# Top-32 attention feeding a gated product on one core: groups of 128 tokens, weights as the moving operand, and the hidden tile turned on TensorE

## The reference, cut to what matters

```
scores = (q @ k.T) / sqrt(64)              # 4 batches, 8 heads, 576 x 576
kth    = 32nd largest of each row
scores = where(scores >= kth, scores, -1e9)
attn   = softmax(scores)                   # sum + 1e-9
x      = (attn @ v) -> [2304 tokens, 512]
out    = ((x @ w_a) * (x @ w_b)) @ w_out   # w_a, w_b: 512 x 1536, w_out: 1536 x 512
```

## Time and profile before

| | |
|---|---|
| median of 3 executions | 875.44 us |
| the profiled execution | 875.8 us, span 874.0 us |
| busy PE, weight loads, DVE, ACT, POOL | 814.9, 734.0, 780.9, 623.4, 455.5 us |
| granted TensorE clock, mean | 0.969 |
| moved by DMA | 81.48 MB, mean 93 GB/s |

### The profile page before, as it was taken

One profiled execution on the slowest core, in us unless ns is written; L12 is line 12 of the kernel. 1 busy time (PEld: TensorE's weight loads), 2 busy tenths in 40 slices (PEclk: granted clock), 3 DMA queues, 4 the chain that ended last, 5 costly groups with the idle time before them and its releaser, 6 DMA issues.

```text
span 874.0 us, 19133 instructions
## 1 busy us (share of the span) xinstructions
PE 814.9 (93%) x6576; PEld 734.0 (84%) x6576; DVE 780.9 (89%) x1663; ACT 623.4 (71%) x1416; POOL 455.5 (52%) x504
## 2 busy tenths in 40 slices
PE   6666679999999999999999999999999999999997
PEld 4455568889899998898899999898999998898996
DVE  7899999998999999999999999999999999995000
ACT  5787777777877777778777777787777777775222
POOL 2677754555544455555554455655445445544332
PEclk9966689999999999999999999999999999999999
DMA  4635552222522232224422322233323222311332
GB/s 124 152 110 164 194 164 56 75 75 75 147 80 68 73 97 74 73 80 128 107 77 73 91 68 74 73 106 89 95 74 103 68 68 68 91 55 56 109 91 85
DMA packets 133520, 81.48 MB, mean 93 GB/s; under 512 B 82736, under 2 KB 110384, under 8 KB 133424
## 3 DMA queue, kind: packets, MB, share of 16 engines
q1 hardware_dynamic: 132880, 80.12, 33.0%
q10 hardware_dynamic: 544, 0.13, 0.1%
HBM read 70.78 MB, written 9.44 MB: 92 GB/s over the span
## 4 chain that ended last, share of the span: by engine, by line
DVE 51%; PE 31%; issue 10%; ACT 4%; POOL 2%; DMA 1%; SPq 0%; ACTq 0%
DVE work L904 25%; DVE best L887 20%; PE ps L536 12%; PE ps L551 6%; DVE keep L919 6%; PE ps L462 3%; PE ps L501 3%; PE ps L484 2%; PE ps L420 2%; POOL scores L810 2%; PE ps L434 1%; ACT scores L670 1%; ACT q_t L635 1%; DMA k_rows_b<-in_k 1%; PE ps L442 0%
## 5 line engine op out<-in xcount | busy, mean ns | idle before, releaser
L887 DVE MAX8 best<-work 128x8 f32<-128x576 f32 x432 | 304.7, 747 | 0.0
L536 PE MATMUL ps<-x_hi,w_hi 128*128 128x256 f32 x864 | 251.4, 291 | 0.9 <-ACT x_lo L688 0.9
L810 POOL TENSOR_TENSOR scores<-scores,keep 128x576 f32<-128x576 f32 x144 | 214.7, 1510 | 58.5 <-DVE keep L919 58.5
L536 PE MATMUL ps<-x_lo,w_hi 128*128 128x256 f32 x864 | 243.2, 281 | 0.0
L904 DVE MATCH_REPLACE8 work<-best,work 128x576 f32<-128x576 f32 x288 | 212.8, 743 | 0.0
L536 PE MATMUL ps<-x_hi,w_lo 128*128 128x256 f32 x648 | 182.4, 281 | 0.0
L536 PEld LDWEIGHTS ps<-x_hi,w_hi 128*128 128x128 f32 x864 | 163.0, 189 | 2.2 <-ACT x_lo L688 1.4
L820 POOL TENSOR_TENSOR h_lo<-ab,h_hi 128x256 fp32r<-128x256 f32 x108 | 81.0, 750 | 158.5 <-ACT h_hi L699 158.5
L536 PEld LDWEIGHTS ps<-x_lo,w_hi 128*128 128x128 f32 x864 | 163.2, 189 | 0.5
L655 ACT ACTIVATE scores<-scores,neg_max 128x576 f32<-128x576 f32 x144 | 111.9, 778 | 68.0 <-POOL scores L810 67.2
L462 PE MATMUL ps<-k_t,q_t 128*128 128x288 f32 x632 | 121.2, 320 | 4.9 <-ACT scores L643 4.9
(11 more groups left out here) (56 smaller groups left out, 1294.4 us busy)
## 6 DMA issues: line engine op xcount, KB each, us to landing
wo_lo<-x_scratch SPq DMA_DIRECT2D x108, 256.0 KB, 2.7
wb_lo<-x_scratch SPq DMA_DIRECT2D x108, 128.0 KB, 2.2
stage<-in_w SPq DMA_DIRECT2D x36, 256.0 KB, 3.0
q_rows<-in_q SPq DMA_DIRECT2D x142, 64.0 KB, 2.3
x_scratch<-wo_lo SPq DMA_DIRECT2D x18, 256.0 KB, 2.8
v_rows<-in_v SPq DMA_DIRECT2D x32, 128.0 KB, 2.4
out<-stage SPq DMA_DIRECT2D x15, 256.0 KB, 2.7
k_rows_a<-in_k SPq DMA_DIRECT2D x16, 128.0 KB, 2.3
```

Of the source, the lines that this page charges most:

```text
L536: last = mm(ps_ab[:, which, :], w, x[:, g % 2, kb, :], start=(kb == 0 and i == 0), stop=(kb == KB - 1 and i == 2))
L810: V.tensor_tensor(row, row, keep[:, j, :], ALU.add).then_inc(mask_done, 1)
L887: ins = V.max(best[:, u % 2, j, 8 * r:8 * r + 8], src)
```

## The change

The group becomes 128 tokens, so there are 18, each with 4 chunks of 384 hidden columns: 72 chunks n, and one of them is started in each slot from slot 5 (n = s - 5), the last slot being 78. x is now stationary and the weights move, 384 columns at a time: 12 matmuls for a and 12 for b, the product with tokens on the partitions. The product of the two therefore has to be turned by PE (`turn_hidden`, three transposes) before it can be the stationary operand of the output. ACT copies the turned h out of PSUM twice, the high part and the whole, and POOL subtracts. In POOL's list the subtraction (`hidden_lo`) of chunk n-2 stands behind the masks and shifts of slot s, that is one slot after the copies. The output product (9 matmuls of 512 columns) is made in two steps, six matmuls from h's high part at the start of the slot, three from its low part later. Each of the two products has a PSUM bank of its own; before, both shared one. The low parts of the output weights are read 768 KB at a time in one buffer, those of w_b 384 KB at a time in one buffer, where before they were in rings of two. The weights are loaded in the order in which the chunks of columns need them, up to five in a slot, through four stages; their outgoing low parts have a tile of their own. The key parts are put in slots 13, 14, 15, 15, 16, 16, 17, 17; 30 to 37; 49, 50, 51, 51, 52, 52, 53, 53; the order of the query tiles changes in two batches, and v is loaded one slot earlier.

```diff
-    G = 256
-    GT = G // P
+    G = P
     GROUPS = TOKENS // G
+    HC = 384
+    HB = HC // P
+    NH = DFF // HC
+    NCH = GROUPS * NH
...
-    ORDER = [[0, 1, 2, 3, 4], [0, 4, 1, 2, 3], [0, 1, 2, 4, 3], [4, 0, 1, 2, 3]]
+    ORDER = [[0, 1, 2, 3, 4], [4, 0, 1, 2, 3], [0, 1, 2, 3, 4], [4, 0, 1, 2, 3]]
...
+        at = first_unit(b, 0)
+        PREP_SLOT += [at + n for n in ((-5, -4, -3, -3, -2, -2, -1, -1) if b % 2 else (-6, -5, -4, -3, -2, -1, 0, 1))]
...
     MOE0 = PER + 1
-    MOE_END = LAST
+    MOE_END = MOE0 + NCH + 2
...
+    STAGES = 4
+    W_AT = [(0, 2), (0, 4)] + [(1, m) for m in (0, 1, 2, 4)] + [(s, m) for s in range(2, 5) for m in range(5)]
+    W_AT += [(s, m) for s in range(5, 9) for m in (0, 1, 2, 4)]
...
+            def load_wo(n):
+                if not 0 <= n < NCH:
+                    return
+                wait(sp, o_done, n)
+                f = n % NH * HB
+                if n < NH:
+                    stored_until(W_ORDER.index(WO0 + f + HB - 1))
+                sp.dma_start(wo_lo[:].bitcast(fp32), xs_o[f * P:(f + HB) * P, :].rearrange("(b p) c -> p b c", p=P)
+                             ).then_inc(ld_wo, 16)
```

SP's loop:

```diff
+            for s in range(FIRST, MOE_END):
...
+                load_wo(n - 1)
+                load_q(s + 4)
+                for b, p in V_AT.get(s, []):
                     load_v(b, p)
+                if n >= 2 and (n - 2) % NH == NH - 1:
+                    store_y((n - 2) // NH)
...
+                load_wb(n + 1)
```

PE's three steps and its loop:

```diff
+            def columns_of(n, which, blocks):
...
+                if which == 0:
+                    wait(pe, xlo_done, PER * g + (3 if blocks[0] == 0 else PER))
+                for kb in blocks:
...
+                    for m, (x, w) in enumerate(((x_hi, high), (x_hi, low), (x_lo, high))):
+                        last = mm(ps_ab[which], x[:, g % 2, kb, :], w,
+                                  start=(kb == 0 and m == 0), stop=(kb == KB - 1 and m == 2))
...
+            def turn_hidden(n):
...
+                pe.wait_ge(h_ready, n + 1)
+                wait(pe, ht_copied, n)
+                for b in range(HB):
+                    last = tr(ps_h[:, b * P:(b + 1) * P], ab[:, 0, b * P:(b + 1) * P], ident[:])
...
+            def output(n, part):
...
+                    if part == 0:
+                        mm(ps_y, h_hi[:, cols], high, start=(f + b == 0), stop=False)
+                        mm(ps_y, h_hi[:, cols], wo_lo[:, b, :], start=False, stop=False)
+                    else:
+                        last = mm(ps_y, h_lo[:, cols], high, start=False, stop=(f + b == NF - 1))
...
+            for s in range(FIRST, MOE_END):
                 mine = preps_at(s)
+                n = s - MOE0
+                output(n - 2, 0)
                 probs_v(s - 2)
                 q_transposes(s + 2)
                 qk(s + 1, 0)
+                columns_of(n, 0, (0, 1))
+                output(n - 2, 1)
                 x_subtract(s - 2)
                 q_subtract(s + 2)
                 qk(s + 1, 1)
                 if mine:
                     wait(pe, qt_ready, min(s + 3, NU))
+                for m in mine:
+                    k_transposes(m)
+                columns_of(n, 0, (2, 3))
+                wait(pe, xlo_done, min(s - 1, NU))
+                turn_hidden(n - 1)
                 wait(pe, qt_ready, min(s + 3, NU))
                 wait(pe, kt_ready, parts_until(s))
                 transposes(s - 1, 0)
+                columns_of(n, 1, (0, 1, 2, 3))
                 transposes(s - 1, 1)
```

The second half of a slot on ACT:

```diff
                 normalise(s - 1, 0)
+                copy_y(n - 2)
                 x_out(s - 2, x_lo, xsub_done, xlo_done)
                 copy_q(s + 2, 1)
                 copy_scores(s + 1, 1)
+                for m in mine:
+                    copy_k(m)
                 normalise(s - 1, 1)
+                copy_hidden(n - 1)
+                weights(s, 2)
+                copy_ab(n, 0)
+                weights(s, 3)
                 copy_probs_t(s - 1, 0)
+                weights(s, 4)
+                copy_ab(n, 1)
                 copy_probs_t(s - 1, 1)
```

A slot on POOL:

```diff
                 masked(s - 1, 0)
                 masked(s - 1, 1)
                 shifts(s)
+                n = s - MOE0
+                hidden_lo(n - 2)
+                hidden(n - 1)
+                for m in range(2, 5):
+                    weights(s - 1, m)
+                weights(s, 0)
+                for m in [m for m in preps_at(s) if not split_early(m)] + [m for m in preps_at(s + 1) if split_early(m)]:
+                    split_k(m)
+                weights(s, 1)
```

More of the change, by code:

```diff
@@ L40, in topk_attention_gated_product @@
     WO0 = 2 * WB0
+    NCB = DFF // WC
     LOW = WO0 - 6
@@ L339, in load_wo @@
[L339 to L352, removed]
@@ L354, in store_y, with load_w @@
-            def store_y(g):
[L355 to L368, removed]
+            def load_w(i):
+                if i < WCH:
+                    wait(sp, w_lo_done, i - STAGES + 1)
+                    sp.dma_start(stage[:, i % STAGES, :], w_parts[W_ORDER[i]]).then_inc(ld_w[i % STAGES], 16)
@@ new lines, in stored_until @@
+            def stored_until(last):
+                for n in range(LOWS):
+                    wait(sp, st_w[n], 16 * sum(LEAVING[m] <= last for m in range(n, len(LEAVING), LOWS)))
+            def load_wo(n):
[7 more added lines that the diff above has]
+                             ).then_inc(ld_wo, 16)
@@ new lines, in load_wb @@
+            def load_wb(n):
+                if not 0 <= n < NCH:
+                    return
+                wait(sp, ab_done[1], n)
+                if n < NH:
+                    stored_until(W_BASE[columns_need(n) - 1] + KB - LKB - 1)
+                at = n % NH * HC
+                sp.dma_start(wb_lo[:].bitcast(fp32), xs_b[:, :, at:at + HC].rearrange("k p c -> p k c")
+                             ).then_inc(ld_wb, 16)
+            def store_y(g):
+                sp.wait_ge(y_ready, g + 1)
+                for at, n, row in PIECES[g]:
+                    sp.dma_start(out[row:row + n, :], y[at:at + n, g % 2, :]).then_inc(st_y, 16)
@@ L375, in _ @@
             load_q(2)
-            for c in range(STAGES):
-                load_w(c)
+            load_w(0)
+            load_w(1)
             load_k(4)
@@ L553, in step @@
+                if part == 1:
                     last.then_inc(o_done, 1)
-            def steps(todo):
-                for n in todo:
-                    step(n)
             pe.wait_ge(s_ident, 2)
@@ new lines, in copy_ab, with copy_hidden @@
+            def copy_ab(n, which):
+                if not 0 <= n < NCH:
+                    return
+                act.wait_ge(ab_done[which], n + 1)
+                if which == 0:
+                    wait(act, ht_done, n)
+                else:
+                    wait(act, h_ready, n)
+                A.copy(ab[:, which, :], ps_ab[which]).then_inc(ab_copied[which], 1)
+            def copy_hidden(n):
+                if not 0 <= n < NCH:
+                    return
+                act.wait_ge(ht_done, n + 1)
+                wait(act, o_done, n)
+                A.copy(h_hi[:], ps_h).then_inc(h_hi_ready, 1)
+                wait(act, h_lo_ready, n)
+                A.copy(h[:], ps_h).then_inc(ht_copied, 1)
```

395 lines of the change are left out of this document (161 added, 234 removed).

## The result

The changed kernel takes 867.5 us in the median (866.3 to 868.4) against 875.4, a ratio of 0.991 [0.989, 0.993]: 7.9 us less. The profiled execution took 866.3 with a span of 864.5. The forecast was 859, so the direction holds and the time lies in the range, but the gain is just under half of the 16.4 that was promised. The kernel before was timed again beside the experiments; its median lay between 874.6 and 875.4, so differences of about 1 us between medians of this document say nothing.

A forecast was written before the change was run, and what follows sets the result against it. The time was taken as the end of DVE's work (D, 798.1 us) plus what PE has left then (75.9). From the profiled 875.8, +5.5 in D and -22.0 behind it gave 859.3, taken as 859; range 847 to 880.

The forecast's parts named there:

- Slot on PE: PE's work in every slot: 10.47 us, 0.24 more than before, 0.09 under DVE's 10.56.
- Distance of matmuls: Start-to-start time of PE's 384-column matmuls: 0.176 us, the midpoint between 0.118 at 256 columns and 0.233 at 512.
- h's path: POOL's low part of h ends 3.8 us into DVE's slot, PE needs it 4.6 into its own: costed at nothing.
- The load: The 768 KB load of `wo_lo` takes 4.7 us: hidden by 0.5 in the slots, not in the tail.
- D: End of DVE's last mask, 798.1 us before: rises 5.5 to 803.6.
- Early slots: Slots 1 to 8, with POOL full in 5 to 8 and PE's clock partly low: adds 4 us (0 to 12).
- Keys: Slots with key parts and neighbours: about 20 have 0.24 less slack on PE, +5 us; 3.5 taken back for `keep`.
- Behind D: What PE has left after DVE's last mask: 53.9 us instead of 75.9, 22.0 less, with load-set slots of 7.9.
- PE as the bound of every slot: Rival: PE stalls exceed the 0.09 slack in each slot; 0.45 per slot costs 24 us, giving 883; chance 0.14.
- The load over 5.3 us: Rival: the `wo_lo` load outlasts its cover in the slots; at 6.2 it adds 60 us, about 919; chance 0.04.
- The gain going to D: Rival: first nine slots +12, keys +12, nothing back; D rises 21 us, time about 875; chance 0.09.
- The collisions of `keep` vanishing: Rival: these and the waits in key slots mostly vanish; D falls 5 us, time 848; chance 0.14.

The follow-up runs named there:

- late inversion: The changed kernel with DVE's inversion a round later, between the two removals of round 2: 866.8 us, ratio 0.991.
- left-out matmuls: The changed kernel without two of each chunk's three output matmuls with h's low part, so part of the product is missing: 849.4 us, ratio 0.973.
- early release: The changed kernel with the next `wo_lo` load issued after the six high output matmuls, not after the three low ones: 859.7 us, ratio 0.983.

## Where the prediction held and where it failed

*Slot on PE, 10.47.* Measured 10.52 in plain slots: matmuls of 384 columns as interpolated, the turn 0.05 longer. So the slack under DVE's 10.56 is 0.04, not 0.09, and in slots with `probs_v` of a 64-row unit (10.59) there is none. Plain slots cost nothing, as forecast.

*Distance of matmuls.* The measured distance at 384 columns, 0.177, is 9% over the 0.163 that the rule on columns over 2.4 GHz gives (the Trainium skill, "TensorE: Matmul & The Clock Gate", section on 56 and 53.3 ns). Going by the rows was right. By that rule the slot would have been 0.5 shorter, not 0.3, since the 9 matmuls of 512 columns count too.

*h's path costs nothing.* Right in the changed kernel: PE waits for `h_lo` nowhere in the slots, and the place behind the masks is worth some 2 us. What I had not seen is the other half of the edit, that the high step covers the copy of the probabilities. I had the output's cost right and its place for granted.

*The load.* 4.7 forecast, 4.7 measured, hidden in the slots and not behind D: right, but for the first three outputs (3.7 us of waits in slots 7 to 9, which no term of mine has).

*D, +5.5 forecast, +8.2 measured.* Early slots: +4 forecast; unit 12 is inverted 2.1 later than before, and the clock that I feared for the first chunk is at 1.00 from 84 us on. Keys: +5 forecast, less 3.5 for `keep`; measured +6.1 from unit 12 to the end. Here is one of the two steps that failed: I took PE's key work and DVE's `keep` as two terms to be added, where a slot is as long as the slower of the two engines needs. From unit 12 to 22 the changed kernel needs 2.3 us more than before, over the third batch's keys (units 29 to 37) 1.1, over the fourth's 2.5.

In the kernel before, the third batch's key slots were not PE's at all:

```profile
358.71 0.15 DVE L914 RECIPROCAL inverse<-sums_eps 128x2 f32<-128x2 f32 x1
...
363.60 1.79 DVE L919 TENSOR_SCALAR keep<-scores,best 128x576 f32<-128x576 f32 x2
...
370.13 0.15 DVE L914 RECIPROCAL inverse<-sums_eps 128x2 f32<-128x2 f32 x1
```

DVE waits for nothing there, and 370.13 - 358.71 = 11.42 is 10.56 plus the 0.85 by which this pair of `keep` exceeds 0.94. Behind unit 12, up to unit 70, the excess of `keep` sums to 10.8 us before and to nothing in the changed kernel. So `keep` gave back three times my 3.5. (My 9 us for all of the excess set a union of intervals, 82.5, against a sum of single durations, 73.6; the sum to compare with is 144 x 0.615 = 88.6.) But DVE's waits over the same units rose from 7.4 to 22.9, because PE is now the slower one in those slots, as the late inversion and the left-out matmuls show. The length of the long slots is PE's work: 10.52, two key parts 0.54 + 0.36 with a switch of 0.09, 1.1 for a unit of 64-row tiles, whose scores are 16 matmuls and not 8, and 0.2 for its four transposes of q instead of two; that makes 12.8. The terms for the 64-row unit were in no sum of mine; in the trace of the changed kernel it is

```profile
202.14 1.23 PE L471 MATMUL ps<-k_t,q_t 128*128 128x288 f32 x8
203.21 0.71 PE L429 MATMUL ps<-ident,k_rows_a 128*128 128x128 f32 x5
203.75 0.60 PE L429 MATMUL ps<-ident,k_rows_b 128*128 128x128 f32 x4
204.11 0.42 PE L546 MATMUL ps<-w_hi,x_hi 128*128 128x384 f32 x1
```

with 203.21 - 202.14 = 1.07 for half of the scores, against 0.52 in a plain slot (645.39 - 644.87, the same timeline). The old kernel had these units too, with 0.33 of slack in the slots around them, and behind unit 12 only three of its slots were over 12 us, against six now. The change also moved key parts and query tiles, so that 64-row units meet pairs of key parts in these six slots; no run put them back, so what that placing costs by itself is not shown.

*Behind D, -22.0 forecast, -17.7 measured.* This is the other step, and the larger, 4.3 us. The mechanism was right, one load and what stands between its landing and the next issue, and the early release shows it; its sizes were not. PE begins slot 72 0.4 late and takes 9.4 for it, not 9.0; slot 73 gives its `o_done` 4.66 in, not 4.41; a slot set by the load is 8.0 to 8.4, not 7.9; and from the first output of chunk 70 to that of 71 it is 7.3, not 6.8. The last wait lets the clock fall, 9 x 0.19 = 1.7 us, which no term had. That the clock would fall behind 4.6 us of idle PE could have been read in the trace of before, where it was at 0.52 in the half-idle stretches.

*The sum.* 2.7 + 4.3 = 7.0, and 859.3 + 7.0 is the profiled 866.3. The median is 1.2 above that.

*Rivals.* PE as the bound of every slot: true in 20 slots and not in the plain ones, where PE stays 0.04 under DVE. The load over 5.3 us: no. The gain going to D: 8.2 of that rival's 21 us did. The collisions of `keep` vanishing: they did, all behind unit 12, but without the fall of D that this rival promised.

## What to carry to other kernels

When two engines nearly tie, cost every kind of slot on both and take the longer, slot by slot; do not add what one loses to what the other gains: slack of one engine that absorbed peaks before is gone after a change that seems to cost it only 0.3 us per slot. And a slot that is long today can be long because of the other engine. A wait total in a table is not a price; move the waiting instruction and see whether the end moves. Before a block of matmuls is merged or moved, look at what another engine does under it; and give a buffer free at its last reader, not at the end of the step that contains it.

## What was unexpected of the hardware

A load of 768 KB landed in 4.7 us and one of 384 KB in 3.3, where 256 KB took 2.7 and 128 KB 2.2: all on or within 0.1 of one line. The fit of the Trainium skill, "DMA: Bandwidth & Descriptors", section on the anatomy of one DMA, gives 3.8 for 768 KB; it is an estimate here, for that fit is of DMAs issued by GpSimd, and these are issued by SyncE. The small loads in the same queue became slower: those of q, 64 KB, landed in 2.3 us in the kernel before and in 4.4 in the changed one (the pages, part 6), and nothing waited for them but PE at the very start.

Three fp32 transposes of 128x128 took 0.32 us to the next start when four more transposes stood behind them (0.36), and 0.25 with columns behind them (822.50 to 822.75, where the first of these then took 0.26 instead of 0.175).
